# Attention masks built from bucket numbers on GpSimd instead of from mask products on TensorE and VectorE, and a two-column sum in place of an added constant

## What is computed

```python
q_bits = (np.einsum('bhsd,dk->bhsk', q, proj) > 0).astype(np.int64)
k_bits = (np.einsum('bhsd,dk->bhsk', k, proj) > 0).astype(np.int64)
powers = 2 ** np.arange(n_bits)                      # n_bits = 6: 64 buckets
q_bucket = np.sum(q_bits * powers, axis=-1)
k_bucket = np.sum(k_bits * powers, axis=-1)
mask = q_bucket[:, :, :, None] == k_bucket[:, :, None, :]
scores = scale * np.matmul(q, k.transpose(0, 1, 3, 2))
scores = np.where(mask, scores, -1000000000.0)
attn = np.exp(scores - np.max(scores, axis=-1, keepdims=True))
attn = attn / (np.sum(attn, axis=-1, keepdims=True) + 1e-09)
return np.matmul(attn, v)
```

## Time and profile before

| | us |
|---|---|
| median of three runs | 770.29 |
| lowest and highest | 770.01 and 770.37 |
| span of the profiled execution, first to last instruction | 767.3 |
| median less span | 3.0 |

### The profile page before, as it was taken

One profiled execution on the slowest core, in us unless ns is written; L12 is line 12 of the kernel. 1 busy time (PEld: TensorE's weight loads), 2 busy tenths in 40 slices (PEclk: granted clock), 3 DMA queues, 4 the chain that ended last, 5 costly groups with the idle time before them and its releaser, 6 DMA issues.

```text
span 767.3 us, 12413 instructions
## 1 busy us (share of the span) xinstructions
PE 716.3 (93%) x3809; PEld 594.8 (78%) x3809; DVE 439.7 (57%) x795; ACT 322.3 (42%) x635; POOL 263.4 (34%) x277
## 2 busy tenths in 40 slices
PE   6899999999999999999999999999937998988995
PEld 2478888888888887888888888888836777777774
DVE  0499999999999965457446446543366211341110
ACT  0087777877777842222212222231224232442221
POOL 1645776677567740035008004400001121131111
PEclk9999999999999999999999999999967999999999
DMA  9722311311331110003001100011045511011010
GB/s 297 237 66 62 79 51 54 92 59 51 92 98 73 48 63 1 0 2 110 0 1 55 55 0 0 1 56 56 0 167 181 215 41 41 27 41 41 28 42 14
DMA packets 22094, 49.84 MB, mean 65 GB/s; under 512 B 3088, under 2 KB 5264, under 8 KB 22064
## 3 DMA queue, kind: packets, MB, share of 16 engines
q1 hardware_dynamic: 19008, 42.34, 16.9%
q0 software_dynamic: 2080, 6.56, 2.5%
q10 hardware_dynamic: 976, 0.56, 0.3%
HBM read 43.16 MB, written 6.55 MB: 65 GB/s over the span
## 4 chain that ended last, share of the span: by engine, by line
PE 77%; DMA 7%; DVE 6%; issue 5%; ACT 2%; POOL 1%; SPq 1%; POOLq 0%; ACTq 0%; DVEq 0%
PE ps L1197 8%; PE ps L1216 7%; PE ps L1361 6%; PE ps L1362 6%; PE ps L1363 6%; PE ps L1343 5%; PE ps L1345 5%; PE ps L1344 5%; DMA x_slot<-y_rows,get_now 4%; PE ps L1230 4%; PE ps L1231 4%; PE ps L1472 3%; PE ps L1474 3%; PE ps L1473 3%; PE ps L1170 2%
## 5 line engine op out<-in xcount | busy, mean ns | idle before, releaser
L621 ACT ACTIVATE probs<-ps,neg_max 128x768 f32<-128x768 f32 x96 | 87.0, 907 | 55.1 <-DVE neg_max L830 55.0
L685 ACT ACTIVATE relu<-ps 128x512 f32<-128x512 f32 x48 | 28.7, 598 | 190.6 <-PE ps L1345 190.6
L839 DVE TENSOR_TENSOR pt_lo<-ps,pt_hi 128x384 fp32r<-128x384 f32 x192 | 98.6, 548 | 5.1 <-ACT pt_hi L632 3.0
L632 ACT ACTIVATE pt_hi<-ps 128x384 fp32r<-128x384 f32 x192 | 86.4, 498 | 25.3 <-PE ps L1216 15.2
L1216 PE MATMUL ps<-cst,probs 128*128 128x128 f32 x576 | 92.2, 277 | 1.7 <-DVE pt_lo L839 0.9
L830 DVE TENSOR_REDUCE neg_max<-ps 128x1 f32<-128x768 f32 x96 | 90.7, 945 | 0.0
L1216 PEld LDWEIGHTS ps<-cst,probs 128*128 128x128 f32 x576 | 69.6, 145 | 10.0 <-DVE pt_lo L839 6.3
L1361 PE MATMUL ps<-wo_hi,g_hi 128*128 128x512 f32 x192 | 76.0, 396 | 0.7 <-DVE xt_lo L907 0.7
L1363 PE MATMUL ps<-wo_hi,g_lo 128*128 128x512 f32 x192 | 75.5, 393 | 0.0
L1362 PE MATMUL ps<-wo_lo,g_hi 128*128 128x512 f32 x192 | 75.4, 393 | 0.0
L1343 PE MATMUL ps<-xt_hi,wi_hi 128*128 128x512 f32 x192 | 75.1, 391 | 0.0
(11 more groups left out here) (159 smaller groups left out, 1500.2 us busy)
## 6 DMA issues: line engine op xcount, KB each, us to landing
w_raw<-w SPq DMA_DIRECT2D x16, 512.0 KB, 6.8
raw_k<-kT SPq DMA_DIRECT2D x32, 192.0 KB, 3.3
raw_q<-qT SPq DMA_DIRECT2D x32, 192.0 KB, 3.5
wi_raw<-w_in SPq DMA_DIRECT2D x4, 1024.0 KB, 5.0
wo_raw<-w_out SPq DMA_DIRECT2D x4, 1024.0 KB, 5.1
pair_raw<-qT SPq DMA_DIRECT2D x8, 384.0 KB, 8.6
pair_raw<-kT SPq DMA_DIRECT2D x8, 384.0 KB, 14.1
raw_v<-v SPq DMA_DIRECT2D x16, 192.0 KB, 2.4
```

Of the source, the lines that this page charges most:

```text
L839: nc.vector.tensor_tensor(pt_lo[c % 2][sl], unit(tt, h).rearrange("p (k q) -> p k q", k=3), pt_hi[c % 2][sl].bitcast(F32), ALU.subtract).t ...
```

## The change

`mask_st`, the six mask products for the next pair and the six stage_mask() of VectorE are gone. In their place, once ahead of the attention, the bucket number of each token is worked out (three products of 256 columns with `powers` for each of q and k, and one VectorE instruction for each, keep_ids()) and stored in HBM as `buckets`, bf16, one row for each head. For each later pair and head SyncE loads that row to 64 partitions (load_buckets()), and GpSimd compares it with the partition's own number `lane`: is_equal and times 2^60 for q, is_equal and minus 1 for k. The product is the same as before. In front of keep_bits(), VectorE has seven small instructions, prepare(), each waited for, among them a product and a sum over 1,024 columns which give the weights in `powers`. Pair 0 still uses mask products and stage_mask(), now named first_mask_of().

`row_sum` has a second column with 1e-9, and add_eps() sums the two columns with a tensor_reduce instead of adding a constant with a tensor_scalar.

```diff
-        row_sum = sb("row_sum", [P, CHUNKS_PER_PAIR, CHUNK_TILES], F32)
+        row_sum = sb("row_sum", [P, CHUNKS_PER_PAIR, CHUNK_TILES, 2], F32)
-        mask_st = sb("mask_st", [P, 2, SEQ], BF16, 2)
+        bucket_of = sb("bucket_of", [P, 2, SEQ], BF16, 2)
+        bucket_ids = sb("bucket_ids", [3 * ID_ROWS, 2, MASK_W], BF16, 2)
+        powers = sb("powers", [NH * NBITS, ID_ROWS], BF16, 2)
...
@@ sync
+            sp.wait_ge(ids_kept, 2)
+            for a in range(3):
+                sp.dma_start(buckets[:, :, MASK_W * a:MASK_W * (a + 1)],
+                             bucket_ids[ID_ROWS * a:ID_ROWS * a + NH, :, :]).then_inc(ids_out, 16)
+            sp.wait_ge(ids_out, 48)
+            def load_buckets(i, z):
+                sp.wait_ge(masks_in, i * 4 + (2 * z - 2))
+                sp.dma_start(bucket_of[half(z, True), :, :], buckets[ds(i * 2 + z, 1), :, :].to_broadcast(
+                    [HD, 2, SEQ])).then_inc(ids_in[z], 16)
             with sp.Fori(1, PAIRS) as i:
-                load_heads(i, False)
+                for z in range(2):
+                    load_head(i, z, False)
+                    load_buckets(i, z)
+                    load_v(i, z, False)
@@ gpsimd, place_masks
-                pool.wait_ge(masks_staged, i * MASK_UNITS + MASK_UNITS)
+                pool.wait_ge(ids_in[z], i * 16)
                 pool.wait_ge(scores_done, i * TILES_PER_PAIR + (QT * (z + 1) - TILES_PER_PAIR))
                 m = half(z, True)
-                for c, stack in ((0, qb), (1, kb)):
-                    copied(stack[z][m, :], mask_st[m, c, :], 1.0, masks_in, i * 4 + (2 * z + c + 1))
+                hold()
+                G.tensor_scalar(qb[z][m, :], bucket_of[m, 0, :], lane[m, :], BIG, ALU.is_equal,
+                                ALU.mult).then_inc(masks_in, 1)
+                pool.wait_ge(masks_in, i * 4 + (2 * z + 1))
+                hold()
+                G.tensor_scalar(kb[z][m, :], bucket_of[m, 1, :], lane[m, :], 1.0, ALU.is_equal,
+                                ALU.subtract).then_inc(masks_in, 1)
+                pool.wait_ge(masks_in, i * 4 + (2 * z + 2))
@@ vector
-                if tt in MASK_TILES and not last:
-                    v_.wait_ge(masks_in, i * 4 + 4)
-                    m = MASK_TILES.index(tt)
-                    stage_mask(m, slice(0, P), mask_st[:, m // 3, :], beside(z, MASK_W)).then_inc(masks_staged, 1)
...
-                nc.vector.tensor_scalar(row_eps[:, c, :], row_sum[:, c, :], 1e-9, None, ALU.add).then_inc(eps_done, 1)
+                nc.vector.tensor_reduce(row_eps[:, c, :], row_sum[:, c, :, :], AX, ALU.add).then_inc(eps_done, 1)
...
+            prepare(nc.vector.memset(row_sum[:, :, :, 1], 1e-9), 1)
+            prepare(nc.vector.memset(powers[:, :], 0.0), 2)
+            prepare(nc.vector.tensor_tensor(weighed, heads, iota128[0:NH * NBITS, 0:HD].unsqueeze(1).to_broadcast(
+                [NH * NBITS, NH, HD]), ALU.mult), 3)
+            weights = x_rows[0:NH * NBITS, 2, 0, 0:NH]
+            prepare(nc.vector.tensor_reduce(weights, weighed, AX, ALU.add), 4)
+            prepare(nc.vector.tensor_copy(powers[:, 0:NH], weights), 5)
+            prepare(nc.vector.tensor_scalar(lane_hi[:, :], tokid[:, 0:1], float(HD), -float(HD), ALU.is_gt, ALU.mult), 6)
+            prepare(nc.vector.scalar_tensor_tensor(lane[:, :], tokid[:, 0:1], -1.0, lane_hi[:, :], ALU.add, ALU.add), 7)
+            def keep_ids(c):
+                v_.wait_ge(ids_turned, c + 1)
+                nc.vector.tensor_scalar(bucket_ids[:, c, :], ps[0:3 * ID_ROWS, 7 - c, 256:512], 1.0 / 32, None,
+                                        ALU.mult).then_inc(ids_kept, 1)
             for c, stack in ((0, qb), (1, kb)):
                 units = range(3 * c, 3 * c + 3)
                 for m in units:
                     keep_bits(m)
+                keep_ids(c)
@@ tensor, first_masks
                     pe.wait_ge(masks_staged, 2)
+                    pe.wait_ge(ids_kept, 1)
                 for m in range(3 * c, 3 * c + 3):
                     pe.wait_ge(bits_done, m + 1)
-                    masks(0, m, first_mask(m)).then_inc(masks_turned, 1)
+                    masks(m, first_mask(m)).then_inc(masks_turned, 1)
+                pe.wait_ge(prepared, 5)
+                for a in range(3):
+                    last_mm = mm(ps[ID_ROWS * a:ID_ROWS * (a + 1), 7 - c, 256:512], powers[:, :],
+                                 bits[:, c, MASK_W * a:MASK_W * (a + 1)], start=True, stop=True)
+                last_mm.then_inc(ids_turned, 1)
@@ tensor, scores
-                if tt in MASK_TILES and not last:
-                    last_mm = masks(i + 1, MASK_TILES.index(tt), beside(tt % 2, MASK_W))
```

More of the change, by code:

```diff
@@ L36 @@
 PIECES = PAIRS // PIECE
-MASK_TILES = (2, 3, 5, 6, 8, 9)
-MASK_UNITS = len(MASK_TILES)
+MASK_UNITS = 6
+ID_ROWS = 32
 BACK_TILES = (10, 1, 4, 7)
@@ L66, in program @@
     y_rows = nc.dram_tensor("y_rows", (TOK, DM), F32).ap()
+    buckets = nc.dram_tensor("buckets", (NH, 2, SEQ), BF16).ap()
     with ExitStack() as ctx:
@@ L123, in program @@
         bits = sb("bits", [NH * NBITS, 2, SEQ], BF16, 2)
-        mask_st = sb("mask_st", [P, 2, SEQ], BF16, 2)
+        bucket_of = sb("bucket_of", [P, 2, SEQ], BF16, 2)
+        bucket_ids = sb("bucket_ids", [3 * ID_ROWS, 2, MASK_W], BF16, 2)
+        powers = sb("powers", [NH * NBITS, ID_ROWS], BF16, 2)
+        lane_hi = sb("lane_hi", [P, 1], F32)
+        lane = sb("lane", [P, 1], F32)
         raw_q = [sb(f"raw_q{z}", [P, SEQ], F32) for z in range(2)]
@@ L263, in program @@
         masks_staged = sem("masks_staged")
+        prepared = sem("prepared")
+        ids_turned = sem("ids_turned")
+        ids_kept = sem("ids_kept")
+        ids_out = sem("ids_out")
+        ids_in = [sem(f"ids_in{z}") for z in range(2)]
         masks_in = sem("masks_in")
@@ L384, in load_v @@
                     "a p t d -> (a p) t d")).then_inc(v_in[z], 16)
[L386 to L389, removed]
             load_head(0, 0, True)
@@ L621, in exp @@
                 nc.scalar.activation(probs[z][:, :], score_bank(z), ACT.Exp, bias=neg_max[:, z:z + 1],
-                                     accum_out=row_sum[:, c, j:j + 1]).then_inc(exp_done, 1)
+                                     accum_out=row_sum[:, c, j, 0:1]).then_inc(exp_done, 1)
             def round_units(i, tt, first):
@@ L804, in keep_bits, with first_mask_of @@
                                         ALU.is_gt).then_inc(bits_done, 1)
-            def stage_mask(m, part, dst, src):
+            def first_mask_of(m, part, dst, src):
                 col = MASK_W * (m % 3)
@@ L813, in stage_mask, with tile_max @@
                                                ALU.is_lt, ALU.mult)
-            def tile_max(i, tt, first, last):
+            def tile_max(i, tt, first):
                 z = tt % 2
                 v_.wait_ge(scores_done, i * TILES_PER_PAIR + (tt + 1))
-                if tt in MASK_TILES and not last:
-                    v_.wait_ge(masks_in, i * 4 + 4)
-                    m = MASK_TILES.index(tt)
-                    stage_mask(m, slice(0, P), mask_st[:, m // 3, :], beside(z, MASK_W)).then_inc(masks_staged, 1)
                 if tt in BACK_TILES:
@@ L862, in pair @@
                     if tt < TILES_PER_PAIR - 1:
-                        tile_max(i, tt + 1, first, last_)
+                        tile_max(i, tt + 1, first)
                     elif not last_:
-                        tile_max(i + 1, 0, False, False)
+                        tile_max(i + 1, 0, False)
                     if tt > 0:
@@ L882, in pair, with prepare @@
                             invert(i - 1, c + CHUNKS_PER_PAIR)
+            def prepare(ins, count):
+                ins.then_inc(prepared, 1)
+                v_.wait_ge(prepared, count)
+            heads = patt[:, :].rearrange("p (h b) -> p h b", b=HD)
+            weighed = x_rows[0:NH * NBITS, 0:2, :, :].rearrange("p a t d -> p (a t d)")[:, 0:NH * HD].rearrange(
+                "p (h b) -> p h b", b=HD)
+            prepare(nc.vector.memset(row_sum[:, :, :, 1], 1e-9), 1)
[11 more added lines that the diff above has]
+                                        ALU.mult).then_inc(ids_kept, 1)
             for c, stack in ((0, qb), (1, kb)):
@@ L891, in _ @@
                         v_.wait_ge(masks_turned, m + 1)
-                        placed = stage_mask(m, half(z, True), stack[z], first_mask(m))
+                        placed = first_mask_of(m, half(z, True), stack[z], first_mask(m))
                         if z == 1:
@@ L898, in _ @@
             nc.vector.memset(ready[:, :], 0.0).then_inc(masks_in, 2)
-            tile_max(0, 0, True, False)
+            tile_max(0, 0, True)
             pair(0, True, False)
@@ L1144, in _, with masks @@
             mm = nc.tensor.matmul
-            def masks(i, m, dst):
-                return mm(dst, patt[:, ds(i * P, P)],
+            def masks(m, dst):
+                return mm(dst, patt[:, 0:P],
```

(11 more changed lines are left out.)

## The result

| | before | changed |
|---|---|---|
| median, us | 770.33 | 795.61 |
| lowest and highest | 770.01 and 773.28 | 792.86 and 797.56 |
| span of the profiled execution | 767.3 | 791.0 |

The ratio is 1.0337, 95% interval 1.0307 to 1.0366. The forecast was 758.5 us, the range 755 to 768.

A forecast was written before the change was run, and what follows sets the result against it. VectorE was taken to set 29.6 us per pair, PE next at 27.6. Gains of 12.1 (six periods), 0.4 (pair 7) and 1.0 (pair 0), 13.5, less 1.7 at the start, gave 11.8 off 770.3: 758.5 us, range 755 to 768.

The forecast's parts named there:

- What bounds the kernel: Attention, per pair: VectorE sets 29.6 us, PE's own work is about 27.6, so VectorE gains are worth at most 2.0.
- Parts 1 and 2: VectorE per pair: six stage_mask() gone, 2.3 us, and add_eps() no longer held by GpSimd, 2.6 us; about 24.7 needed.
- rival A: The new add_eps() reduction is held by GpSimd as before; 8 us gained, 762 us; chance 0.12.
- Part 3: GpSimd's four compares per pair take 0.82 us each; d longer costs max(0, 2d - 1.3) + max(0, 2d - 1.7) per pair.
- rival C: GpSimd's compares are slow outright, kernel slower than before; at 2.9 us each 25 us slower, 795 us; chance 0.13.
- Rival B: GpSimd becomes the bound in part, with compares of 1.5 to 1.95 us; 760 to 767 us; chance 0.15.
- Part 4: Ahead of the attention: bucket products, prepare() and keep_ids() on the path cost 1.7 us, bounds 1.4 and 2.8.
- the middle case: prepare() ahead of keep_bits() is done at 24.0 us, its product having waited for GpSimd's instruction ending just ahead of 20.99.
- (b): Start: prepare() delays keep_bits(), mostly covered by 1.9 us before PE wants its result; cost taken as 0.3 us.
- (a): Start: three products with `powers` for q stand amid the projection, which keeps PE busy; cost 0.4 us.
- (c): Start: for k, three more products, then keep_ids(), stand in series ahead of the staging; cost 1.0 us.
- sign of a falling clock: Start: PE's clock falling once more in the longer start was named as a sign that the prediction is wrong.

## Why the prediction was wrong, step by step

**What bounds the kernel: right.** VectorE at 29.6, PE's own work close behind. With the sum alone the period is 28.32 against 28.3 worked out; with copies for compares it is 27.90, where the forecast took 27.6 within 27.3 to 28.0. The three tiles of pair 7 were a good model of pair 7 (27.66 with copies), and 0.2 short of a looped pair. The two kernels together price the six mask products at no more than 28.32 - 27.90 = 0.4 us per pair, not 0.7.

**Parts 1 and 2: right.** VectorE's busy time is 24.64 against 24.7. The reduction is never held by GpSimd (0.149 us in 32 of 32), so rival A is out. By the Trainium skill, SBUF — State Buffer, section "SBUF: two separate sides", this was to be expected, and the runs agree. What the prediction took from there as well, that the one waits for the other's end, they bear out for GpSimd's copies and two-input instructions and not for its slow compare, as shown above.

**Part 3: the step that failed.** It said of the compare "I take 0.82, the same instruction but for the operators". The operators are what matters: 2.86 us. Of the two rows that I took for bounds neither bounds it. The two-input instruction at 1.83 us was no upper end, and "even two inputs take 1.83", my argument against rival C, has no force. With the right duration the working stands: d = 2.04 gives 2 x 4.08 - 3.0 = 5.2 us per pair, measured 5.4, and rival C at "2.9 us" gave 795 us, measured 795.6. That it took 2.9 for its example was luck, since no row gave it, and its two terms are each a little large: the seven periods take 195.1 us with copies, so the compares cost 230.5 - 195.1 = 35.4 us, not 37, and the rest of the change saved 205.7 - 195.1 = 10.7 there (from unrounded times), where the forecast had 12.5. So the mechanism and its price were on record, and the chance of 0.13 and the range's end at 768 were the error. (Rival B's top is also summed wrong: by the formula a compare of 1.95 us gives 769, not 767.) The trace gave a hint that I passed over: all of GpSimd's tensor_scalar in it are one form, multiply by multiply, though for a copy one operation would do. A trace that knows one form only says nothing about another.

**The estimate of 1.5 us.** The Trainium skill, GPSIMD Engine Reference, section "Performance pitfalls for Q7 kernels", led to an estimate of 1.5 us for the compare. The runs don't bear it out: a lone compare takes 2.14 us, and a lone multiply, which gives no truth value, 2.13.

**Part 4: right, term by term.** The first score tile came 1.5 us later than in the kernel before (forecast 1.7). That alone says little, since the start spreads by more from trace to trace, but its parts can be read one by one. In the changed kernel VectorE ahead of the attention reads:

```profile
20.53 1.35 DVE L915 TENSOR_TENSOR x_rows<-patt,cst 96x1024 f32<-96x1024 bf16 x1
20.98 2.58 POOL L512 TENSOR_TENSOR kb<-raw_k,ka 64x768 fp32r<-64x768 f32 x1 [0.18 <-POOL qa L508]
...
24.00 1.08 DVE L828 TENSOR_SCALAR bits<-ps 96x256 bf16<-96x256 f32 x3
```

keep_bits() began at 24.00. That is the time of the middle case, by luck: the product didn't wait for GpSimd, the last constant landed at 20.18 in place of 19.7 and the copy into `powers` took 0.42 us. PE's mask products began at 25.22 against 25.10: (b) is 0.1, forecast 0.3. With copies, where PE had run at full clock and was earlier, PE waited 0.79 us for keep_bits(), so (b) hangs on the stage ahead of it. From q's mask products to k's it is 9.23 us against 8.84: (a) is 0.4, as forecast. From k's to the first score tile it is 2.98 against 1.96: (c) is 1.0, as forecast. The HBM round trip was hidden: GpSimd's first split_qk of pair 1 waited for PE's scores, not for a load. Two small things besides. The sign of a falling clock came true: it was 0.50 in tile 0 of pair 0 and 0.70 in tile 1, where the kernel before had 1.00 (and 0.50 later, in tile 3); pair 0 still took 21.7 us from its first score tile to tile 11 against 23.4, a gain of 1.7 where the sum had 1.0. And the 3.0 us that the sum puts around the span are the median less the span of another execution; in every run on record the time is 1.8 to 1.9 above its own span. The forecast starts from the median, so nothing hangs on it.

## What to carry to other kernels

Before work is moved to an engine, ask whether the trace has that instruction with those operations on that engine. The size and kind of the operands are not enough: on GpSimd the pair of operators alone made 0.83 or 2.8 us here. Then compare what the engine has to spare per round (here 2.8 us) with what it gets (8.1). And a gain on the engine that sets the pace is worth measuring alone: here one line gave 1.1%, and the larger change around it hid that.

## What the runs showed that I had not expected

- GpSimd's tensor_scalar is fast for multiply-multiply and multiply-add only; all the others that were tried, even a lone multiply, take 2.6 to 3.4 times as long. For the compare that is by the element; for the others it was not tried. The Trainium skill, GPSIMD Engine Reference, section "When to use GPSIMD", calls one-input work there roughly line-rate; of what was tried that can hold for the fast pairs alone.
- VectorE can hold GpSimd too: GpSimd's instruction of 20.98 above took 2.58 us, 1.80 before, while VectorE's product with two SBUF inputs ran from 20.53 to 21.88. Ten traces have this pair of instructions: where VectorE's began first, in seven, GpSimd's took 2.57 to 2.77; where GpSimd's began first, in three, it took 1.80 and VectorE's 1.90 to 2.87 in place of 1.22.
- TensorE's clock fell in the changed kernel after the longer waits, and it cost nothing that shows. PE waited 2.8 to 2.9 us at tile 0 of pairs 2 to 7; in five of these six the granted clock was 0.57 to 0.74 from there to tile 1, in pair 5 it was 1.00. Tile 0 to tile 1 after waits of 2.8 to 2.9 us, changed kernel, with the columns of the earlier trace rows (the clock is third from the end):

```profile
95.29:98.86 3.57, 3.57 (x14) 3.38 (x15) 1.59 (x3) 1.09 (x3) 2.86 (x3) 0.58 0.29 87
190.00:195.11 5.11, 2.31 (x17) 1.94 (x15) 3.24 (x7) 3.51 (x8) 4.77 (x2) 1.00 0.53 154
195.11:197.29 2.18, 2.18 (x15) 2.09 (x16) 1.17 (x2) 0.84 (x3) 1.53 (x2) 1.00 0.23 86
```

At 95.29 the granted clock is 0.58, near the lower of TensorE's two levels, 1.2 GHz of 2.4, and the tile takes 3.57 us; at 195.11 it is full, and the tile takes 2.18. The periods around them are 33.37 and 33.26: PE simply waits 0.96 us at tile 6 in the first and 2.32 in the second. As long as GpSimd sets the pace, PE's slower clock fills a wait that would be there anyway. Why pair 5 was spared, these rows don't tell.
